# Order of the first gates, memsets and input transfers in a gated-attention and two-expert-layer kernel

## What is computed

```
for t in range(768):                                    # q, k, v: (4, 8, 768, 40)
    m_new = max(f[t] + m, i[t])
    C = exp(f[t]+m-m_new) * C + exp(i[t]-m_new) * outer(v[t], k[t])
    n = exp(f[t]+m-m_new) * n + exp(i[t]-m_new) * k[t]
    y[t] = sigmoid(o[t]) * (C @ q[t]) / max(|n . q[t]|, 1)
x = y as (3072, 320)
e = argmax(x @ w_gate);  x = p[e] * (relu(x @ w1[e]) @ w2[e])    # 8 experts, 320 -> 1024 -> 320
h = x @ w_in;  out = max(0.01*h, h) @ w_out                      # 320 -> 2048 -> 320
```

## Time and profile before

| what | value |
|---|---|
| median of 3 runs | 857.47 us |
| lowest and highest | 855.05 and 863.86 us |
| time of the profiled execution | 860.35 us |
| its span, first to last instruction | 858.6 us |
| mean granted TensorE clock | 0.969 |
| PE, DVE, ACT, POOL busy | 754.0, 535.2, 391.2, 146.7 us |
| moved by DMA | 99.75 MB |

### The profile page before, as it was taken

How to read it: one execution, slowest core, us unless ns; L and a number is a source line. 1 busy time by engine, 2 the same in 40 slices (tenths; PEclk the granted TensorE clock), 3 DMA queues, 4 the chain that set the end, 5 groups by cost and what they waited for, 6 DMA issues and landing times.

```text
span 858.6 us, 17692 instructions
## 1 busy us (share of the span) xinstructions
PE 754.0 (88%) x6435; PEld 553.7 (64%) x6436; DVE 535.2 (62%) x1406; ACT 391.2 (46%) x713; POOL 146.7 (17%) x202
## 2 busy tenths in 40 slices
PE   0789999998278899999999899999999999999993
PEld 0577887886167788888888755555555555555552
DVE  6468998896957556765567745455455454454341
ACT  2457474572526366554546233343433433434331
POOL 4334343443031111111100000010100100100101
PEclk9999999999589899999999999999999999999998
DMA  9569999991063983679420000000000000000000
GB/s 237 136 163 304 286 302 304 272 236 60 0 197 140 358 294 111 232 256 349 136 73 2 2 1 1 1 32 1 23 9 1 31 0 0 31 0 1 32 1 31
DMA packets 49401, 99.75 MB, mean 116 GB/s; under 512 B 7822, under 2 KB 38222, under 8 KB 46766
## 3 DMA queue, kind: packets, MB, share of 16 engines
q1 hardware_dynamic: 39906, 67.65, 26.4%
q10 hardware_dynamic: 6780, 22.10, 7.5%
q0 software_dynamic: 2640, 9.01, 3.1%
HBM read 74.85 MB, written 23.89 MB: 115 GB/s over the span
## 4 chain that ended last, share of the span: by engine, by line
PE 69%; DVE 12%; issue 7%; DMA 4%; ACT 4%; SPq 1%; POOL 1%; DVEq 0%; ACTq 0%
PE bank L1514 26%; PE bank L1649 13%; PE bank L1548 11%; PE bank L1381 4%; PE bank L1410 4%; ACT stage L856 2%; DVE qk L1320 2%; DMA vv<-v_in 2%; PE bank L1402 1%; PE bank L1394 1%; PE bank L1433 1%; DMA d_parts<-xreg 1%; DVE stage L1315 1%; DVE sxt L1295 1%; PE bank L1504 1%
## 5 line engine op out<-in xcount | busy, mean ns | idle before, releaser
L1514 PE MATMUL bank<-stage,slot 128*128 128x512 f16 x768 | 181.3, 379 | 0.0
L1649 PE MATMUL bank<-slot,dec 128*128 128x320 f16 x768 | 159.3, 299 | 15.7 <-DVE qk L1320 13.0
L1514 PE MATMUL bank<-qbd,slot 128*128 128x128 f16 x1984 | 122.3, 225 | 11.9 <-issue 11.7
L1315 DVE TENSOR_TENSOR stage<-bank,stage 128x512 f32<-128x512 f32 x96 | 66.4, 692 | 105.2 <-ACT stage L856 98.3
L1514 PEld LDWEIGHTS bank<-qbd,slot 128*128 128x128 f16 x1984 | 118.2, 101 | 15.4 <-issue 15.0
L1514 PEld LDWEIGHTS bank<-stage,slot 128*128 128x128 f16 x768 | 75.2, 98 | 74.1
L856 ACT ACTIVATE stage<-bank 128x512 f32<-128x512 f32 x96 | 57.5, 599 | 128.6 <-PE bank L1514 126.9
L1649 PEld LDWEIGHTS bank<-slot,dec 128*128 128x128 f16 x768 | 73.0, 98 | 66.9 <-DVE qk L1320 23.7
L1649 PE MATMUL bank<-slot,qk 128*128 128x320 f16 x384 | 114.8, 299 | 0.0
L1548 PE MATMUL bank<-slot,emov 128*128 128x320 f16 x496 | 102.0, 299 | 2.3 <-issue 1.5
L1320 DVE TENSOR_TENSOR qk<-stage,dec 128x512 f16<-128x512 f32 x96 | 66.3, 691 | 52.1 <-ACT dec L860 52.1
(11 more groups left out here) (261 smaller groups left out, 1133.5 us busy)
## 6 DMA issues: line engine op xcount, KB each, us to landing
slot<-d_w SPq DMA_DIRECT2D x12, 1280.0 KB, 6.7
d_w<-slot ACTq DMA_DIRECT2D x4, 2560.0 KB, 9.8
stage<-wB SPq DMA_DIRECT2D x6, 1280.0 KB
stage<-wA SPq DMA_DIRECT2D x6, 1024.0 KB
d_w<-slot SPq DMA_DIRECT2D x4, 1280.0 KB, 8.3
stage<-wB ACTq DMA_DIRECT2D x4, 1280.0 KB
qk<-qkT SPq DMA_DIRECT2D x12, 360.0 KB
slot<-qkT SPq DMA_DIRECT2D x12, 360.0 KB
```

What stands on the lines that cost most here:

```text
L1315: v.tensor_tensor(fgl[f % 2], bank[f % 2][:, :], ft[f % 2], ALU.max).then_inc(f_g, 1)
L1514: ins = t_.matmul(pf, a[:, col:col + P], x(k), start=(q == 0), stop=(q == len(ops) - 1))
L1649: ins = t_.matmul(bank[4 + q][:, 0:DM], x[f % 2][:, q * P:(q + 1) * P], slotB[2 + f // NF][:, c0:c0 + DM], start=(f == 0 and z == 0), stop ...
```

## The change

On DVE, only the first 128 columns of `gr0` are set ahead of the gate chain. The four memsets of `esta` follow the parts of the first positions, and after them the rest of `gr0`. A new count `GATE_SETS` marks the end of the `esta` memsets: ACT waits for it before it reads the parts back (`esta` rows 3 to 5 are written by that), and POOL waits for it before `late_set(2)`.

On SP, o of b = 0 and 1 is asked for after q, k, v of both. Then SP waits for the eighth transfer of b = 1 (its parts read back), asks for the inputs of b = 2, `load_A(2)`, o of b = 2, the inputs of b = 3, the router weights, and last `load_B(2)`. The wait for `parts_stored` is gone. All tables of the weights move by one step (units 2, 3, 0, 1 and 4).

```diff
             for b in range(2):
                 load_k(0, b)
-                load_o(0, b)
                 sp.wait_ge(set_done, SETS[b])
                 load_q(0, b)
                 load_v(0, b)
-            load_A(2)
-            load_B(2)
+            for b in range(2):
+                load_o(0, b)
+            sp.wait_ge(in_landed[1], landed(0, 1))
+            for b in range(2, B):
+                load_k(0, b)
+                sp.wait_ge(set_done, SETS[b])
+                load_q(0, b)
+                load_v(0, b)
+                load_e(0, b)
+                if b == 2:
+                    load_A(2)
+                load_o(0, b)
             sp.wait_ge(act_const, 6)
             ... router weights ...
-            sp.wait_ge(parts_stored, 16)
-            for b in range(2, B):
-                load_k(0, b)
-                load_o(0, b)
-                sp.wait_ge(set_done, SETS[b])
-                load_q(0, b)
-                load_v(0, b)
-                load_e(0, b)
+            load_B(2)
...
+            pool.wait_ge(gate_chain, GATE_SETS)
             late_set(2)
...
             act.wait_ge(set_done, SETS[1])
+            act.wait_ge(gate_chain, GATE_SETS)
             act.wait_ge(parts_stored, 16)
...
-            link(v.memset(gr0, 1.0))
+            link(v.memset(gr0[:, 0:P], 1.0))
             link(v.memset(gm0[:, 0:1], NEG))
-            for i in range(2):
-                link(v.memset(esta[i][:, :].bitcast(F32), 0.0))
-                link(v.memset(esta[i][0:3, :].bitcast(F32), TWO_ONES))
...
             parts(gp0[:, 0:3, :], gM, -1.0, 0, P)
             parts(gp0[:, 3:6, :], gb, 1.0, 0, P)
+            for i in range(2):
+                link(v.memset(esta[i][:, :].bitcast(F32), 0.0))
+                link(v.memset(esta[i][0:3, :].bitcast(F32), TWO_ONES))
+            link(v.memset(gr0[:, P:S], 1.0))
...
-SUMS_AT = {3: 2, 7: 3, 12: 0, 17: 1, 22: 4}
-LOAD_A = {2: 3, 8: 0, 13: 1, 18: 4}
-LOAD_B = {3: 3, 9: 0, 14: 1, 19: 4}
-STORE_A = {6: 2, 11: 3}
-STORE_B = {8: 2, 13: 3}
+SUMS_AT = {4: 2, 8: 3, 13: 0, 18: 1, 23: 4}
+LOAD_A = {3: 3, 9: 0, 14: 1, 19: 4}
+LOAD_B = {4: 3, 10: 0, 15: 1, 20: 4}
+STORE_A = {7: 2, 12: 3}
+STORE_B = {9: 2, 14: 3}
```

More of the change, by code:

```diff
@@ L921, in _ @@
             assert n[0] == GATE_PARTS, n[0]
+            for i in range(2):
+                link(v.memset(esta[i][:, :].bitcast(F32), 0.0))
+                link(v.memset(esta[i][0:3, :].bitcast(F32), TWO_ONES))
+            assert n[0] == GATE_SETS, n[0]
+            link(v.memset(gr0[:, P:S], 1.0))
             for c in range(1, NC):
@@ L1690 @@
 TWO_ONES = 1.0019378662109375
-GATE_FIRST = 6 + 5
+GATE_FIRST = 2 + 5
 GATE_PARTS = GATE_FIRST + 8
-GATE_SCAN = GATE_PARTS + NC - 1 + 1 + 2 * (NC - 1) + 1
+GATE_SETS = GATE_PARTS + 4
+GATE_SCAN = GATE_SETS + 1 + NC - 1 + 1 + 2 * (NC - 1) + 1
 GATE_ALL = GATE_SCAN + 8
@@ L1711 @@
 SLOT = (0, 1, 0, 1, 2, 3, 2, 3, 2, 3)
-SQUARES = {(1, 2): (2, 0), (1, 3): (2, 1), (2, 0): (2, 2), (2, 2): (2, 3), (2, 3): (2, 4),
[4 rows of a table removed]
-HIGHS = {(4, 0): (2, 0), (4, 3): (2, 1), (5, 0): (2, 2), (6, 0): (2, 3), (7, 0): (2, 4),
[3 rows of a table removed]
-LOWS = {(4, 2): (2, 0), (5, 0): (2, 1), (5, 2): (2, 2), (6, 2): (2, 3), (7, 2): (2, 4),
[3 rows of a table removed]
-SUMS_AT = {3: 2, 7: 3, 12: 0, 17: 1, 22: 4}
-LOAD_A = {2: 3, 8: 0, 13: 1, 18: 4}
-LOAD_B = {3: 3, 9: 0, 14: 1, 19: 4}
-STORE_A = {6: 2, 11: 3}
-STORE_B = {8: 2, 13: 3}
+SQUARES = {(2, 0): (2, 0), (2, 2): (2, 1), (2, 3): (2, 2), (3, 0): (2, 3), (3, 2): (2, 4),
[4 rows of a table added]
+HIGHS = {(5, 0): (2, 0), (5, 3): (2, 1), (6, 0): (2, 2), (7, 0): (2, 3), (8, 0): (2, 4),
[3 rows of a table added]
+LOWS = {(5, 2): (2, 0), (6, 0): (2, 1), (6, 2): (2, 2), (7, 2): (2, 3), (8, 2): (2, 4),
[3 rows of a table added]
+SUMS_AT = {4: 2, 8: 3, 13: 0, 18: 1, 23: 4}
[3 more added lines that the diff above has]
+STORE_B = {9: 2, 14: 3}
 PAIR_SQ = {1: ((5, 0), (5, 1), (5, 2)), 2: ((5, 3), (5, 4)), 6: ((6, 0), (6, 1), (6, 2)), 7: ((6, 3), (6, 4)),
```

## The result

The median went from 857.25 us (20 runs) to 852.04 us (20 runs). The ratio is 0.9942, with a 95% interval of 0.9923 to 0.9961, so 5 us gained. Forecast was 844.5 us, within 840 to 853: the gain forecast, 13.0 us, was 2.5 times what came.

A forecast was written before the change was run, and what follows sets the result against it. PE was taken as busy nearly everywhere, so only its idle time at the start and in steps 4 to 6 could be won: 11.2 - 1.4 + 3.8 - 0.6 = 13.0 us, median 857.5 to 844.5, range 840 to 853.

The forecast's parts named there:

- The start: Stretch before step 0: 0.9 memsets, 1.5 POOL, 5.3 store, 3.5 readback; step 0 begins 11.2 us earlier.
- the 0.9 for the memsets: Gate chain on DVE: with memsets behind the parts, the scan starts at 3.6 instead of 4.49, gain 0.9 us.
- the 1.5 for POOL: Gate chain on DVE: with POOL held back, the 1.84 us cast should be 0.21; 1.5 taken, bounds 0 and 1.6.
- some 3 us of traffic remain: First store of the gate parts: takes 4.0 us beside remaining traffic, landing at 12.0 instead of 19.64.
- The rival of the slow store: First store: its 9.27 us are the price of 192 small pieces beside any full queue; 856.5 us, chance 0.09.
- Rest of the gates: Store on SP's queue before step 4: lands at 37.5, not 35; stall 1.4 us, bounds 0 and 5.
- The 285 GB/s of the forecast: Rate for SP's 5.64 MB until step 4: 19.8 us, until 36.5; at 259 GB/s until 38.5.
- Steps 4 to 7: Waits before steps 5 and 6, with the step's hold, shrink: 3.8 us gained, 13.6 us counted at step 7.
- Steps 8 to 23: Same work, weights one step later; DMA queue has 3% of 106 us to spare: 0.6 us taken off.
- DMA erodes it: Unit 2's 2.9 MB move into the free 17.6 us; queue paces steps 5 to 8; 7 us gained, 850.5, chance 0.22.
- the offset is under 9 by step 8: Sign of the erosion rival: step 0 starts early but the offset is under 9 by step 8.
- The tail: Unit 4's scale moves from the gap between steps 22 and 23 into the tail: 1.4 out, 1.4 in.

The follow-up runs named there:

- changed_again: The changed kernel unaltered, timed and traced a second time: 850.93 us, ratio 0.9935.
- changed_third: The changed kernel unaltered, timed and traced a third time: 849.55 us, ratio 0.9895.
- e10: Changed kernel with both stores of the gates' rest on ACT's queue and the twelve broadcasts ahead of SP's wait for the parts: 848.12 us, ratio 0.9883.
- relieved_again: The code of e10 timed and traced a second time: 847.11 us, ratio 0.9879.
- relieved_gates_back: The code of e10 with the memsets of DVE and POOL back ahead of the gate chain: 846.13 us, ratio 0.9861.
- e1: The kernel before with only the change's edits of DVE, ACT and POOL, SP's order and tables as before: 855.15 us, ratio 0.9981.
- before_again: The kernel before unaltered, a second trace: attention ends at 212.4 us; no median or ratio is given.
- no_broadcasts: The changed kernel without the twelve broadcasts of the decays and DVE's wait on them: 852.43 us in one run, no ratio.

## Why the prediction was right and wrong

**The start: right in sum, wrong in its parts.** 11.2 us were forecast for step 0 and 10.95 came (10.6 to 11.9 over the traces). But of the four terms, the 0.9 for the memsets and the 1.5 for POOL are worth nothing; that the sum came out was luck. The store left when I said, 2.2 us earlier than before, and waited all of it out behind SP's inputs. I had written that "some 3 us of traffic remain", and yet added an earlier issue to a landing that this traffic sets. A store that leaves into a queue with a fixed drain time gains nothing by leaving early. The rival of the slow store fell: 1.7 to 5.6 us, not 9.3. (The prediction's "slices 4 to 10" for DMA should read 4 to 9: the tenth digit of the earlier trace rows is a 1.)

**Rest of the gates: the mechanism right, the size off.** Forecast was a store behind 4 us of backlog, 1.4 us of stall. In the trace the store left 2.7 us later than said, because SP's own issue had stalled: 6.26 us for three q transfers. It took 7.08 us instead of 5, and DVE waited 5.92 (4.08 and 6.16 in the other traces) instead of 0.9 to 2.3. I had worked out the backlog and counted it for the store, but not for the issue of everything between. The kernel before shows the like where its router weights follow the 2.8 MB of unit 2, timeline of its SP queue:

```profile
10.03 4.57 SPq L381 DMA_DIRECT2D xw<-wg_in  x3
```

The 285 GB/s of the forecast stands in no row. While the queue was full, from 17 to 38, it moved 261 GB/s in the changed kernel's first trace and 270 in its second, close to the second value of the forecast, 259.

**Steps 4 to 7: the term that failed.** 3.8 us more were to be gained there, by unit 3's A and B coming behind the inputs. Against the forecast's lead of 13.6 at step 7, the traces have 5.5, 7.4 and 5.5. The first `exponents` of each step on PE:

| step | before | forecast | changed | changed_again | changed_third | e10 |
|---|---|---|---|---|---|---|
| 4 | 54.1 | 44.3 | 45.2 | 43.7 | 45.0 | 44.2 |
| 5 | 63.8 | 51.2 | 55.1 | 54.1 | 55.0 | 51.5 |
| 6 | 73.0 | 59.0 | 65.6 | 64.0 | 65.6 | 60.1 |
| 7 | 79.9 | 65.9 | 74.4 | 72.5 | 74.4 | 68.6 |

Step 4 began within 1 us of the forecast. Step 5 came 3 to 4 us late, behind DVE's wait for the broadcasts in step 4, and steps 6 and 7 by another 4 to 5, of which 2.45 + 1.00 us are PE's waits for their inputs in the first trace. SP came to that point 5 us later than I had it (48.5 for 43.2), so A was asked for when it always had been, DMA was busy for only 0.47 of the time from 38 to 55, and the inputs of steps 6 and 7 were late again. The sum treated the queue's capacity as given from 43 us on, and that capacity went unused because the issuer was not there. e10 shows the term: with SP there in time, steps 4 and 5 begin within 0.3 us of the forecast and step 6 1.1 late; the lead at step 7 is 11.3 (10.8 in relieved_again, 12.1 in relieved_gates_back), and still not 13.6, with waits of 0.65 and 0.66 us for the inputs of steps 6 and 7.

**Steps 8 to 23.** Taken at -0.6. In the changed kernel's three traces the lead moved by -0.6, +1.1 and +0.3 us between step 7 and the last `turn`, so this term is about right. With the chain relieved, the lead ends at 6.8 to 11.1 across three traces, and without o's loads it grows from 12.5 at step 7 to 15.4: the share of 0.97 meant a queue near its limit, where a lead did not grow of itself and other waits came and went between executions. My rival "DMA erodes it" (0.22) named the sign rightly, "the offset is under 9 by step 8", the store's delay (4.8 us for its 4) and nearly the price (850.5 us; 852.04 came). Its mechanism was only partly so. The early mix did run at 240 GB/s in the window 15 to 38, but at a share of 0.94, and e10 has 254 GB/s there and keeps its lead; steps 5 to 7 were not paced by a full queue, since DMA was half idle from 38 to 55. What made them late is the chain on SP.

**The tail** was neutral as said. From the `turn` in step 21 on, three intervals follow: 8.3, 8.3 and 6.9 us in the kernel before, 6.9, 8.3 and 8.4 in the changed one. The scale of unit 4 has moved from the first to the last of them.

## What to carry over

When a start moves forward, follow the issuing queue instruction by instruction to the next place where it waits for a landing: if it meets that place at the same clock time as before, the gain ends there. A free DMA queue is only worth what someone is there to put into it, and behind it, where the share was 0.97, the changed kernel won next to nothing of its lost lead back. Before adding up gains on a path to a transfer's landing, ask whether its issue or the queue ahead of it sets the landing.

## What was unexpected of the hardware

A backlog of transfers slows the issuer too: three transfers of q took SP 6.26 us to issue behind unit 2's B, with some 2 MB still outstanding (an estimate: 5.0 MB asked for since 15.8, less 12 us at 235 GB/s), and 1.18 in a quiet queue. Small stores are held up whatever queue they come from: 0.24 MB took 6.1 and 6.9 us from ACT's queue and 7.1 from SP's, against 2.45 in the quiet, and 48 KB took 1.7 us where almost nothing was left ahead and 10.49 in e1.

A store from ACT's queue is not held for all that SP asked for before it. In before_again SP asks for unit 2's B at 9.41 and ACT's store goes out at 10.86; transfers issued there, KB and us to landing:

```profile
stage<-wB SPq DMA_DIRECT2D x1, 1280.0 KB, 14.4
...
d_parts<-xreg ACTq DMA_DIRECT2D x1, 48.0 KB, 9.0
```

So the store landed near 19.9 and B near 23.8. Whether transfers asked for after a store delay it as well is not shown: in e1 1.8 of unit 2's 2.8 MB were asked for after it and it landed 5 us later than in the changed kernel, but the 1.0 MB asked for just before it make 4 of these at 259 GB/s (an estimate). The Trainium skill, page "DMA: Bandwidth & Descriptors", section "Queues, rings and completion order", says that an engine takes turns between queues. before_again agrees with that: the store took 9.0 us beside SP's traffic, against 1.7 where that had drained, but it did not wait for the whole backlog.

The time behind attention, which the change does not touch, varied by 6.5 us between executions (642.7 to 649.2 from the last turn to the end). A 30 us stretch of the first pairs, from 60 us behind the last turn, shows what may be one part of it: the granted clock was 0.89 in one trace of the changed kernel and 0.97 in another. First changed_third, then the changed kernel:

```profile
266.10:296.10 30.00, 25.45 (x292) 22.13 (x289) 18.22 (x43) 12.35 (x20) 4.35 (x4) 0.89 1.01 360
```

```profile
267.00:297.00 30.00, 26.51 (x327) 22.67 (x325) 19.24 (x42) 14.52 (x23) 4.08 (x3) 0.97 1.01 362
```

A clock between the two levels is a mean over the stretch. In it PE did 327 products at the higher mean and 292 at the lower. The clock is not all of it: no_broadcasts, with the longest time behind attention, had a clock of 1.00 in the same stretch, with a DMA share of 0.83. I had set the sum against one profiled execution, as if its 860.35 us were fixed.
